# A fused attention and two-layer expert kernel: weights prepared once and kept in memory, gate column sums as products, low parts of x on two engines

## The chip, the cores and the metric

The kernel runs on one core of a Trainium2 chip. The core has a matrix engine (PE, with its weight loads shown apart as PEld), a vector engine (DVE), an activation engine (ACT), a general engine (POOL), and a queue engine (SP) that here issues every DMA. Each engine works through its own list of instructions in order; they meet only in semaphores. The metric is the device time of one execution in microseconds, lower is better.

## The reference, cut to what matters

```python
# 1: attention, 4 batches x 8 heads x 768 tokens x 64; each chunk of 32 queries sees its own
#    keys, 16 before, 8 behind and 8 memory keys        -> x: 3072 tokens x 512
# 2: first layer
a = x @ w_a                       # 512 -> 1536
b = x @ w_b
x = (a * b) @ w_out               # 1536 -> 512
# 3: gated experts, E = 8
logits = x @ w_gate
P = np.exp(logits - logits.max())
for _ in range(8):
    P /= P.sum(1, keepdims=True) + 1e-09      # rows: the 8 experts of one token
    P /= P.sum(0, keepdims=True) + 1e-09      # columns: all 3072 tokens of one expert
    P *= N / E
for e in range(E):
    h = np.maximum(x @ w1[e], 0.0)            # 512 -> 1024
    out += P[:, e:e+1] * (h @ w2[e])          # 1024 -> 512
```

All in float32. The kernel forms each float32 product of the two layers from three products of a coarse format (fp32r): every operand is split in a high part and a low part (what is left over).

## The kernel before, in words

**Stages.** Attention comes first. Then the first layer runs in 18 units (`v`, `M1 = 18`), and the expert layer in 96 units (`u`, `M2 = 96`). The tokens are cut into three pairs of token blocks (`PAIRS = 3`, 1024 tokens each). A pair takes `V1 = 6` units of the first layer or `V2 = 32` units of the expert layer, one unit for each slice of 256 hidden columns. So each weight slice is used by three units, one for each pair.

**A unit.** A chain is one "up" product x @ w for one slice; it is computed by a seven-product scheme on 2x2 blocks (`up(c, pos)`, pos 0 to 6, six matmuls each: two halves of the contraction times three high/low combinations). A unit of the first layer has two chains (w_a, w_b), a unit of the expert layer one. Between the up products PE works on the eight `down(w - 1, g)` groups, six matmuls each, of the unit before. So a unit of the first layer has 132 matmuls of 128x512, one of the expert layer 90.

**Weights.** For each unit SP loads a raw slice of 512 KB for each chain and one for down (`load_up`, `load_down`) into one of two slots of `raw`, as soon as the low parts of the slice before in that slot are done. POOL forms the sums of the scheme (`up_sums`, four instructions), ACT writes the high parts (`up_hi`, `down_hi`), POOL the low parts (`up_lo`, `down_lo`) into `W1` and `W2`, which have two buffers each. PE waits for the low parts (`w1_lo`, `w2_lo`) at pos 0 and at g 0. This is done again for every pair, 3 times for each slice.

**The operand x.** The seven left operands of a pair stand in `X`, one buffer. While the last chain of a pair runs, each is rebuilt for the next pair as its product gets done: `operand_sum` on DVE (four differences of 128x1024, in place in `Y`), `operand_hi` on ACT, `operand_lo` on POOL, in the order `X_BUILD`. There are five such changes of operand behind the first build: in units v = 5, v = 11, v = 17 (to the expert layer), u = 31 and u = 63. In the first layer POOL also forms the low parts of the hidden values (`g_lo`, four in each unit).

**The gate.** The logits of all tokens are collected in `gate` (128 x 24 x 8). The maximum and the eight rounds of the normalisation run in units u = 1 to 4: DVE does the row part and the column part (`sinkhorn_round`, `sinkhorn_columns`, each instruction waiting for the one before it, `link`), POOL adds over the partitions in between with `partition_all_reduce`. DVE runs three rounds in a row early in each of u = 2, 3, 4 (`sinkhorn_slot`), among its `accumulate` calls, which free the three PSUM banks of down (PE waits for `y_acc`). At the end of u = 4 `scale_first` multiplies the first expert's results by the gate.

The order on every engine is written out by hand. The code that the change touches:

## Time and profile before

| | us |
|---|---|
| median of 3 runs | 2885.74 (2880.82 to 2885.99) |
| the profiled execution, its device time | 2885.65 |
| its span, first to last instruction | 2883.9 |
| DVE busy | 1386.6 (48%) |
| ACT busy | 1051.4 (36%) |
| POOL busy | 1565.5 (54%) |
| DMA | 160.47 MB, mean 56 GB/s |

Times are in us unless marked ns. L12 is line 12 of the kernel. A row of the timeline gives start, duration, engine, line, operation, output <- inputs, count, and in brackets the idle time of that engine just before and what ended it ("issue": nothing that the profile shows). PEclk, the third number from the end in a row of a window, is the granted clock of PE as a share of 2.4 GHz; behind it stand the mean busy share of the 16 DMA engines and what they moved in GB/s. A busy PE is not a PE at its peak: at half the clock its matmuls last twice as long and it is still busy.

### The profile page before, as it was taken

How to read it: one execution, taken by the hardware profiler on the slowest of the kernel's cores; microseconds unless marked ns; L12 is line 12 of the kernel's file. 1: busy time of each engine (PE TensorE's matmuls, PEld its weight loads, DVE VectorE, ACT ScalarE, POOL GpSimd, SP SyncE). 2: the span in 40 equal slices, each digit the busy share in tenths (PEclk: the TensorE clock that was granted, in tenths of full speed). 3: DMA queues.
4: the chain of work that ended last, by engine and by line, in shares of the span. 5: the costliest groups of instructions: out<-in, count | busy, mean ns of one | idle time of the engine just before them, and what ended most of it. 6: DMA issues, size and time to landing. Idle time of an engine off the chain costs nothing.

```text
span 2883.9 us, 34150 instructions
## 1 busy us (share of the span) xinstructions
PE 2800.7 (97%) x12750; PEld 2263.1 (78%) x12750; DVE 1386.6 (48%) x1969; ACT 1051.4 (36%) x2149; POOL 1565.5 (54%) x1379
## 2 busy tenths in 40 slices
PE   9999989989986899999999999999999999999999
PEld 7877867867865788888887888888887888888887
DVE  4553343343355645444445545454545545454544
ACT  5664333333331233333333333333334333333332
POOL 3358786686773444454547445444547454454542
PEclk8989999999997999999999999999999999999999
DMA  7541111111110111111111211111111211111111
GB/s 133 118 95 47 58 41 46 52 44 45 52 44 29 44 47 56 45 59 45 59 45 55 77 51 52 48 56 45 58 44 52 81 52 52 51 52 49 54 45 51
DMA packets 196940, 160.47 MB, mean 56 GB/s; under 512 B 96944, under 2 KB 164528, under 8 KB 196784
## 3 DMA queue, kind: packets, MB, share of 16 engines
q1 hardware_dynamic: 196784, 158.38, 18.5%
q8 instruction: 99, 1.62, 0.2%
q14 instruction: 57, 0.47, 0.1%
HBM read 152.06 MB, written 6.29 MB: 55 GB/s over the span
## 4 chain that ended last, share of the span: by engine, by line
PE 90%; DVE 4%; POOL 3%; issue 3%; ACT 1%; DMA 0%; POOLq 0%; ACTq 0%; DVEq 0%
PE bank L536 41%; PE bank L603 41%; PE bank L476 2%; PE bank L498 2%; POOL X L383 1%; PE bank L487 1%; PE bank L472 1%; POOL W L372 1%; PE bank L456 1%; DVE Y L930 0%; PE bank L462 0%; POOL hid L402 0%; DVE Y L1056 0%; DVE Y L1002 0%; DVE Y L936 0%
## 5 line engine op out<-in xcount | busy, mean ns | idle before, releaser
L536 PE MATMUL bank<-X,W 128*128 128x512 f32 x5550 | 1430.3, 396 | 40.7 <-POOL X L383 20.4
L536 PEld LDWEIGHTS bank<-X,W 128*128 128x128 f32 x5550 | 1046.9, 189 | 295.7 <-POOL X L383 23.6
L603 PE MATMUL bank<-W,hid 128*128 128x512 f32 x4608 | 1176.0, 394 | 27.7 <-DVE Y L1002 26.7
L603 PEld LDWEIGHTS bank<-W,hid 128*128 128x128 f32 x4608 | 870.2, 189 | 227.1 <-DVE Y L1002 28.0
L999 DVE SCALAR_TENSOR_TENSOR Y<-bank,gate,Y 128x512 f32<-128x512 f32 x720 | 540.4, 751 | 607.2 <-PE bank L603 595.3
L377 POOL TENSOR_TENSOR W<-raw,W 128x1024 fp32r<-128x1024 f32 x114 | 276.0, 2421 | 541.5 <-ACT W L731 541.5
L372 POOL TENSOR_TENSOR W<-Ws,W 128x512 fp32r<-128x512 f32 x264 | 337.8, 1301 | 68.0 <-ACT W L723 68.0
L361 POOL TENSOR_TENSOR Ws<-raw 128x256 f32<-128x256 f32 x132 | 101.2, 767 | 358.4 <-DMA raw<-in_moe_w_dram 320.6
L372 POOL TENSOR_TENSOR W<-raw,W 128x512 fp32r<-128x512 f32 (+1 forms) x264 | 263.7, 1019 | 16.3 <-ACT W L723 16.3
L837 ACT ACTIVATE hid<-tmp 128x512 fp32r<-128x512 f32 x192 | 121.4, 632 | 400.7 <-DVE tmp L967 277.7
L603 PE MATMUL bank<-hid,W 128*128 128x512 f32 x864 | 225.3, 397 | 3.9 <-issue 3.8
L1102 DVE SCALAR_TENSOR_TENSOR hid<-bank,hid 128x512 fp32r<-128x512 f32 x192 | 132.7, 691 | 154.9 <-ACT hid L837 154.5
L781 ACT ACTIVATE tmp<-bank 128x512 f32<-128x512 f32 x132 | 78.5, 595 | 333.1 <-PE bank L536 333.0
L603 PEld LDWEIGHTS bank<-hid,W 128*128 128x128 f32 x864 | 164.7, 191 | 42.5 <-issue 5.6
L1002 DVE TENSOR_TENSOR Y<-Y,bank 128x512 f32<-128x512 f32 x144 | 98.7, 685 | 206.6 <-PE bank L603 206.3
L777 ACT ACTIVATE bank<-bank 128x512 f32<-128x512 f32 x131 | 76.2, 582 | 324.3 <-PE bank L536 324.3
L723 ACT ACTIVATE W<-Ws 128x512 fp32r<-128x512 f32 x264 | 151.1, 623 | 80.8 <-POOL Ws L366 80.8
L962 DVE TENSOR_TENSOR tmp<-bank,tmp 128x512 f32<-128x512 f32 x132 | 91.2, 691 | 180.3 <-ACT tmp L785 180.3
L837 ACT ACTIVATE hid<-bank 128x512 fp32r<-128x512 f32 x192 | 114.5, 596 | 164.5 <-PE bank L536 164.5
L785 ACT ACTIVATE tmp<-bank 128x512 f32<-128x512 f32 x132 | 78.8, 597 | 249.2 <-PE bank L536 249.2
L1102 DVE SCALAR_TENSOR_TENSOR hid<-tmp,hid 128x512 fp32r<-128x512 f32 x192 | 157.7, 821 | 5.3 <-ACT hid L837 1.7
L402 POOL TENSOR_TENSOR hid<-tmp,hid 128x512 fp32r<-128x512 f32 x72 | 97.8, 1361 | 99.8 <-ACT hid L791 99.2
(80 smaller groups left out, 1866.4 us busy)
## 6 DMA issues: line engine op xcount, KB each, us to landing
raw<-in_moe_w_dram SPq DMA_DIRECT2D x192, 512.0 KB, 3.4
raw<-in_moe_w_a_dram SPq DMA_DIRECT2D x18, 512.0 KB, 3.6
raw<-in_moe_w_b_dram SPq DMA_DIRECT2D x18, 512.0 KB, 3.5
raw<-in_moe_w_out_dram SPq DMA_DIRECT2D x18, 512.0 KB, 3.3
Kw<-in_k_dram SPq DMA_DIRECT2D x32, 240.0 KB
Vw<-in_v_dram SPq DMA_DIRECT2D x32, 240.0 KB
Qw<-in_q_dram SPq DMA_DIRECT2D x32, 192.0 KB
out_dram<-Y SPq DMA_DIRECT2D x24, 256.0 KB, 4.0
```

Source lines behind the costliest of these rows:

```text
L361: nc.gpsimd.tensor_tensor(s1, w_block(slot, 1, 0), w_block(slot, 1, 1), ALU.add).then_inc(w_sum, 1)
L372: nc.gpsimd.tensor_tensor(w_piece(c, n, 1), w_piece_of(slot, n), w_piece(c, n, 0).bitcast(F32), ALU.subtract).then_inc(w1_lo, 1)
L377: nc.gpsimd.tensor_tensor(W2[:, w % 2, 1, :], raw[:, item_w2(w) % 2, :], W2[:, w % 2, 0, :].bitcast(F32), ALU.subtract).then_inc(w2_lo, 1)
L402: nc.gpsimd.tensor_tensor(hid[:, v % 2, f, l, 1], g_of, hid[:, v % 2, f, l, 0].bitcast(F32), ALU.subtract).then_inc(f_lo, 1)
L536: last = nc.tensor.matmul(into[:, :], W1[:, c % 2, ws, w_slot, kc, :], X[:, pos, xs, kc, :], start=(start and kc == 0 and n == 0), stop=(k ...
L603: last = nc.tensor.matmul(into[:, :], lhsT, rhs, start=(j == 0 and n == 0), stop=(j == 1 and n == 2))
L723: nc.scalar.activation(w_piece(c, n, 0), w_piece_of(slot, n), ACT.Copy).then_inc(w1_hi, 1)
L837: nc.scalar.activation(hid[:, u % 2, f, l, 0], of, ACT.Relu).then_inc(e_hi, 1)
L962: nc.vector.tensor_tensor(into, bank[BANK_E][:, :], of, ALU.add).then_inc(c_22, 1)
L999: nc.vector.scalar_tensor_tensor(out=y, in0=ps, scalar=by, in1=y, op0=ALU.mult, op1=ALU.add).then_inc(y_acc, 1)
L1002: nc.vector.tensor_tensor(y, y, ps, ALU.add).then_inc(y_acc, 1)
L1102: nc.vector.scalar_tensor_tensor(out=hid[:, u % 2, f, l, 1], in0=of, scalar=0.0, in1=hid[:, u % 2, f, l, 0].bitcast(F32), op0=ALU.max, op1 ...
```

## The change

Weights: the units of the first pair of each layer (`fresh(w)`) prepare their weights as before, and SP stores the finished `W1` (1.84 MB) and `W2` (1.05 MB) buffers in two DRAM tensors (`keep_up`, `keep_down`). The units of the other two pairs load them from there straight into `W1` and `W2` (`fetch_up`, `fetch_down`). Of 36 + 96 chains 12 + 32 are still prepared.

```diff
+        w1_kept = nc.dram_tensor("w1_kept", [2 * V1 + V2, P, 4 * NP * P], F32).ap()
+        w2_kept = nc.dram_tensor("w2_kept", [V1 + V2, P, 4 * D], F32).ap()
+            def keep_up(c):
+                sp.wait_ge(w1_lo, 4 * (kept_w1(c) + 1))
+                sp.dma_start(w1_kept[kept_w1(c)], W1[:, c % 2]...).then_inc(s_w1s[c % 2], 16)
+            def keep_down(w):
+                sp.wait_ge(w2_lo, kept_w2(w) + 1)
+                sp.dma_start(w2_kept[kept_w2(w)], W2[:, w % 2]...).then_inc(s_w2s[w % 2], 16)
+            def fetch_up(c):
+                sp.wait_ge(p_prod, NP * (c - 1))
+                sp.wait_ge(s_w1s[c % 2], 16 * (V1 if c < C1 else V1 + V2 // 2))
+                sp.dma_start(W1[:, c % 2]..., w1_kept[kept_w1(c)]).then_inc(s_w1l[c % 2], 16)
+            def fetch_down(w):
+                sp.wait_ge(p_down, NG * (w - 1))
+                sp.wait_ge(s_w2s[w % 2], 16 * (V1 // 2 if w < M1 else V1 // 2 + V2 // 2))
+                sp.dma_start(W2[:, w % 2]..., w2_kept[kept_w2(w)]).then_inc(s_w2l[w % 2], 16)
             load_down(0)
-            for w in range(1, M1):
+            keep_up(0)
+            for w in range(1, V1):
                 load_up(2 * w)
+                keep_up(2 * w - 1)
                 load_up(2 * w + 1)
+                keep_down(w - 1)
                 load_down(w)
-            for u in range(M2):
+                keep_up(2 * w)
+            load_up(C1)
+            keep_up(2 * V1 - 1)
+            load_down(M1)
+            keep_down(V1 - 1)
+            for w in range(V1, M1):
+                fetch_up(2 * w)
+                fetch_up(2 * w + 1)
+                fetch_down(w)
+            keep_up(C1)
+            for u in range(1, V2):
                 load_up(C1 + u)
+                keep_down(M1 + u - 1)
                 load_down(M1 + u)
-                if u % V2 == 3 and u >= V2:
+                keep_up(C1 + u)
+            keep_down(M1 + V2 - 1)
+            for u in range(V2, M2):
+                fetch_up(C1 + u)
+                fetch_down(M1 + u)
+                if u % V2 == 3:
                     store(u // V2 - 1)
```

PE waits for `s_w1l`, `s_w2l` instead of `w1_lo`, `w2_lo` in those units. ACT's `up_hi` and `down_hi` wait also for the store of the buffer that they write over.

Low parts: DVE takes those of x for pos 3 and 5 and all of `g_lo`; POOL keeps pos 0, 1, 2, 4, 6. ACT's order of the high parts becomes 0, 1, 3, 2, 4, 5, 6. POOL's list is now: weights of v = 0 to 5, the three operand changes of the first layer with the weights of C1 before the third, weights of u = 0 to 31, two operand changes.

```diff
-X_BUILD = (0, 3, 1, 4, 2, 5, 6)
+X_POOL = (0, 1, 2, 4, 6)
+X_DVE = (3, 5)
+X_HI = (0, 1, 3, 2, 4, 5, 6)
+            def operand_lo(n, p, pos):                 # on DVE
+                dve.wait_ge(x_hi, NP * n + X_HI.index(pos) + 1)
+                nc.vector.tensor_tensor(X[:, pos, 1], x_source(p, pos), X[:, pos, 0].bitcast(F32),
+                                        ALU.subtract).then_inc(x_lo2, 1)
+            def g_lo(v, n, f, l):                      # on DVE
+                dve.wait_ge(f_hi, 4 * v + n + 1)
...
                 accumulate(v - 1, 4)                   # DVE, first layer
+                if n is not None:
+                    operand_sum(n, of, 1)
                 dve.wait_ge(f_a, 2 * v + 1)
                 dve.wait_ge(p_prod, NP * b + 4)
                 times(v, 0, bank[BANK_A][:, :])
+                if n is not None:
+                    operand_sum(n, of, 3)
                 accumulate(v - 1, 5)
-                    operand_sum(n, (p + 1) % PAIRS, 0)
-                    operand_sum(n, (p + 1) % PAIRS, 1)
+                g_lo(v, 0, 0, 0)
...
                 times(v, 2, bank[BANK_B][:, :])
+                g_lo(v, 1, 1, 1)
+                if n is not None:
+                    operand_sum(n, of, 2)
                 accumulate(v - 1, 7)
+                g_lo(v, 2, 0, 1)
                 sum_21(b, tmp[:, 4], tmp[:, 4])
                 dve.wait_ge(c_21, b + 1)
                 times(v, 3, tmp[:, 4])
...
-                    operand_sum(n, (p + 1) % PAIRS, 2)
-                    operand_sum(n, (p + 1) % PAIRS, 3)
+                    operand_lo(n, of, 3)
+                g_lo(v, 3, 1, 0)
+                if n is not None:
+                    operand_sum(n, of, 4)
+                    operand_lo(n, of, 5)
                 seed(c)                                # ACT, first layer, second chain
-                up_hi(c + 1)
+                if n is not None:
+                    operand_hi(n, of, 0, c)
+                if fresh(v + 1):
+                    up_hi(c + 1)
                 act.wait_ge(c_21, c)
                 copy_u(c, tmp[:, 4])
...
                 g_hi(v, 0, 0, 0)
+                if n is not None:
+                    operand_hi(n, of, 1, c)
                 act.wait_ge(c_22, c)
                 copy_v(c, tmp[:, 5])
...
                 g_hi(v, 3, 1, 0)
                 if n is not None:
-                    for x in range(3, NP):
-                        operand_hi(n, (p + 1) % PAIRS, x, c)
+                    operand_hi(n, of, 4, c)
+                    operand_hi(n, of, 5, c)
+                    operand_hi(n, of, 6, c)
```

Gate: the reductions over the partitions are products on PE into bank 6, a column of ones times the sums, and the maxima times a unit matrix. DVE's slots are spread over the unit, and PE takes the products after fixed groups of its own list. The column part has three instructions instead of four.

```diff
+            TOTALS = [(u, pos) for u in range(2, 6) for pos in (1, 3, 6)][1:1 + SINKHORN]
+            def total(n):
+                pe.wait_ge(g_one, 1)
+                pe.wait_ge(g_part, n + 1)
+                nc.tensor.matmul(b_sum[:, 0:E], one.to_broadcast([P, P]), col_s, start=True,
+                                 stop=True).then_inc(g_total, 1)
                     down(w - 1, pos)                   # PE, in the loop over pos
+                    if u == 1 and pos == 6:
+                        spread_maxima()
+                    if (u, pos) in TOTALS:
+                        total(TOTALS.index((u, pos)))
-                        nc.gpsimd.partition_all_reduce(col_t[:, :], col_s[:, :], P, RADD).then_inc(g_total, 1)
             def sinkhorn_columns(i):
-                dve.wait_ge(g_total, i + 1)
-                link(nc.vector.tensor_scalar(col_t[:, :], col_t[:, :], EPS, None, ALU.add))
-                link(nc.vector.reciprocal(col_t[:, :], col_t[:, :]))
-                link(nc.vector.tensor_scalar(col_t[:, :], col_t[:, :], float(N) / E, None, ALU.mult))
+                dve.wait_ge(g_total, i + 2)
+                link(nc.vector.tensor_scalar(col_t, b_sum[:, 0:E], EPS, float(E) / N, ALU.add, ALU.mult))
+                link(nc.vector.reciprocal(col_t, col_t))
                 link(nc.vector.tensor_tensor(by_expert, by_expert, ...))
+                slots = [3 * (u - 2) + g for g in range(3)] if u in (2, 3, 4) else [SINKHORN + 1] * 3
                 accumulate(w - 1, 0)
                 accumulate(w - 1, 1)
+                sinkhorn_slot(slots[0])
...
                 h_lo(u, 1, tmp[:, v_at], 1, 1)
+                sinkhorn_slot(slots[1])
...
                 accumulate(w - 1, 7)
+                sinkhorn_slot(slots[2])
```

## Rows read from the trace of the kernel before

**Rows 1.** The page: busy time, share and instructions of each engine.
```profile
PE 2800.7 (97%) x12750; PEld 2263.1 (78%) x12750; DVE 1386.6 (48%) x1969; ACT 1051.4 (36%) x2149; POOL 1565.5 (54%) x1379
```
**Rows 2.** Windows: from:to, length, busy of PE, PEld, DVE, ACT, POOL; PEclk, DMA, GB/s.
```profile
259.07:350.48 91.41, 91.41 (x397) 74.11 (x397) 32.73 (x48) 35.38 (x63) 66.73 (x63) 1.00 0.17 52
350.48:430.26 79.78, 67.69 (x265) 53.19 (x265) 32.68 (x36) 30.44 (x49) 64.14 (x50) 0.91 0.13 40
586.65:635.08 48.43, 36.99 (x133) 28.19 (x133) 22.30 (x20) 18.54 (x28) 41.51 (x29) 0.86 0.10 33
805.07:837.53 32.46, 23.19 (x91) 17.66 (x90) 20.23 (x19) 12.87 (x19) 29.23 (x18) 0.95 0.06 17
862.37:988.31 125.94, 94.32 (x361) 73.03 (x360) 78.22 (x139) 28.08 (x49) 48.16 (x49) 0.84 0.10 34
988.47:1506.64 518.17, 518.17 (x2252) 422.29 (x2251) 257.09 (x350) 176.52 (x300) 256.28 (x225) 1.00 0.16 51
1506.64:1553.30 46.66, 43.49 (x181) 34.69 (x181) 28.16 (x32) 20.45 (x31) 34.40 (x21) 0.96 0.11 34
2175.10:2221.81 46.71, 43.55 (x181) 34.77 (x181) 28.24 (x32) 20.45 (x31) 34.45 (x21) 0.96 0.10 34
```
**Rows 3.** Timeline of unit u = 2 and 3, where the gate is normalised.
```profile
890.64 0.43 POOL L444 PARTITION_ALL_REDUCE col_t<-col_s  x1 [6.80 <-issue]
891.10 0.17 DVE L1039 TENSOR_SCALAR col_t<-col_t 128x8 f32<-128x8 f32 x1 [19.57 <-POOL col_t L444]
894.03 0.68 DVE L1002 TENSOR_TENSOR Y<-Y,bank 128x512 f32<-128x512 f32 x1
894.22 0.40 POOL L444 PARTITION_ALL_REDUCE col_t<-col_s  x1 [3.15 <-DVE col_s L1035]
894.76 2.93 PE L603 MATMUL bank<-W,hid 128*128 128x512 f32 x6 [13.80 <-DVE Y L1002]
...
909.43 2.09 DVE L1039 TENSOR_SCALAR col_t<-col_t 128x8 f32<-128x8 f32 x1
917.46 0.69 DVE L1002 TENSOR_TENSOR Y<-Y,bank 128x512 f32<-128x512 f32 x1
```
**Rows 4.** Timeline of the same stretch, the fold of the logits.
```profile
857.32 0.95 PE L625 MATMUL bank<-fold,lg 128*128 128x8 f32 x8
```
**Rows 5.** Timeline of the operand change in v = 5, and one sum before it.
```profile
203.85 1.21 DVE L936 TENSOR_TENSOR Y<-Y 128x1024 f32<-128x1024 f32 x1
...
388.42 1.05 ACT L751 ACTIVATE X<-Y 128x1024 fp32r<-128x1024 f32 x1
...
390.42 2.41 POOL L383 TENSOR_TENSOR X<-Y,X 128x1024 fp32r<-128x1024 f32 x1
...
392.86 2.30 DVE L930 TENSOR_TENSOR Y<-Y 128x1024 f32<-128x1024 f32 x1 [1.56 <-POOL X L383]
...
395.19 3.27 DVE L933 TENSOR_TENSOR Y<-Y 128x1024 f32<-128x1024 f32 x1
...
413.73 5.49 PE L536 MATMUL bank<-X,W 128*128 128x512 f32 x12 [6.13 <-POOL X L383]
```
**Rows 6.** Timeline of one steady unit of the expert layer, its weights.
```profile
1077.17 2.42 POOL L377 TENSOR_TENSOR W<-raw,W 128x1024 fp32r<-128x1024 f32 x1 [6.08 <-ACT W L731]
...
1079.61 0.37 SPq L280 DMA_DIRECT2D raw<-in_moe_w_dram  x1
...
1084.91 0.37 SPq L273 DMA_DIRECT2D raw<-in_moe_w_dram  x1
...
1088.47 0.74 POOL L361 TENSOR_TENSOR Ws<-raw 128x256 f32<-128x256 f32 x1 [3.59 <-DMA raw<-in_moe_w_dram]
...
1091.13 0.74 POOL L366 TENSOR_TENSOR Ws<-raw,Ws 128x256 f32<-128x256 f32 x1
```
**Rows 7.** Windows: the attention stage; the stretch with eight output stores and two loads.
```profile
0.00:200.00 200.00, 195.72 (x1456) 157.46 (x1457) 99.05 (x203) 116.47 (x538) 77.93 (x91) 0.92 0.59 119
1583.30:1593.30 10.00, 10.00 (x45) 8.16 (x44) 4.97 (x7) 4.06 (x7) 3.44 (x4) 1.00 0.93 316
```

More of the change, by code:

```diff
@@ L113, in build @@
         b_lg, b_gate = bank[6], bank[7]
+        b_sum = bank[6]
         s_kq = [sem(f"s_kq{i}") for i in range(2)]
@@ L139, in build @@
         w2_lo = sem("w2_lo")
+        s_w1s = [sem(f"s_w1s{i}") for i in range(2)]
+        s_w2s = [sem(f"s_w2s{i}") for i in range(2)]
+        s_w1l = [sem(f"s_w1l{i}") for i in range(2)]
+        s_w2l = [sem(f"s_w2l{i}") for i in range(2)]
         x_sum = sem("x_sum")
@@ L207, in w_piece_of, with fresh, unit_of_chain, kept_w1 @@
             return Ws[:, 2 * n - 4:2 * n - 2].rearrange("p s c f -> p (s c) f")
+        def fresh(w):
+            return w < V1 or M1 <= w < M1 + V2
+        def unit_of_chain(c):
+            return c // 2 if c < C1 else M1 + c - C1
+        def kept_w1(c):
+            return c % (2 * V1) if c < C1 else 2 * V1 + (c - C1) % V2
+        def kept_w2(w):
+            return w % V1 if w < M1 else V1 + (w - M1) % V2
+        def loads_w1(c):
+            return sum(not fresh(unit_of_chain(i)) for i in range(c % 2, c + 1, 2))
+        def loads_w2(w):
+            return sum(not fresh(i) for i in range(w % 2, w + 1, 2))
         def item_w1(c):
-            return 3 * (c // 2) + c % 2 if c < C1 else 3 * M1 + 2 * (c - C1)
+            return 3 * (c // 2) + c % 2 if c < C1 else 3 * V1 + 2 * (c - C1)
         def item_w2(w):
-            return 3 * w + 2 if w < M1 else 3 * M1 + 2 * (w - M1) + 1
+            return 3 * w + 2 if w < M1 else 3 * V1 + 2 * (w - M1) + 1
         def unit_of(w):
@@ L396, in _ @@
                     up_lo(0)
-            operand_lo(0, 0, 6)
-            def g_lo(v, n, f, l):
-                pool.wait_ge(f_hi, 4 * v + n + 1)
-                g_of = tmp[:, n]
-                nc.gpsimd.tensor_tensor(hid[:, v % 2, f, l, 1], g_of, hid[:, v % 2, f, l, 0].bitcast(F32),
-                                        ALU.subtract).then_inc(f_lo, 1)
-            for v in range(M1):
-                p, i = unit_of(v)
+            operand_lo(0, 0, 4)
+            for v in range(V1):
                 up_sums(2 * v + 1)
@@ L542, in operands_ready @@
             def operands_ready(c, pos, n):
-                if pos == 0:
-                    pe.wait_ge(w1_lo, 4 * (c + 1))
-                if n is not None:
-                    pe.wait_ge(x_lo, NP * n + X_BUILD.index(pos) + 1)
+                if pos == 0 and fresh(unit_of_chain(c)):
+                    pe.wait_ge(w1_lo, 4 * (kept_w1(c) + 1))
+                elif pos == 0:
+                    pe.wait_ge(s_w1l[c % 2], 16 * loads_w1(c))
+                if n is not None and pos in X_POOL:
+                    pe.wait_ge(x_lo, len(X_POOL) * n + X_POOL.index(pos) + 1)
+                elif n is not None:
+                    pe.wait_ge(x_lo2, len(X_DVE) * n + X_DVE.index(pos) + 1)
             def up(c, pos, n):
@@ L581, in down @@
                 i = NG * w + g
-                if g == 0:
-                    pe.wait_ge(w2_lo, w + 1)
+                if g == 0 and fresh(w):
+                    pe.wait_ge(w2_lo, kept_w2(w) + 1)
+                elif g == 0:
+                    pe.wait_ge(s_w2l[w % 2], 16 * loads_w2(w))
                 if g % 4 == 0:
@@ L627, in gates_fold, with spread_maxima @@
                 last.then_inc(g_mm, 1)
+            def spread_maxima():
+                pe.wait_ge(g_max, 1)
+                nc.tensor.matmul(b_sum[:, 0:P], col_s[:, 0:1].to_broadcast([P, P]), ident[:, :],
+                                 start=True, stop=True).then_inc(g_total, 1)
+            def total(n):
[3 more added lines that the diff above has]
+                                 stop=True).then_inc(g_total, 1)
             pe.wait_ge(a_kt, R)
@@ L760, in _ @@
                 attention_step((B - 1) * G + g, g, G, ahead=(g < G - 1))
-                if g != 2:
-                    operand_hi(0, 0, (0, 1, 3, 4, 5, 6, 7).index(g), None)
                 if g == 2:
                     up_hi(0)
+                for pos in ((0,), (), (), (1,), (3,), (), (2, 4), (5, 6))[g]:
+                    operand_hi(0, 0, pos, None)
             for g in range(3):
@@ L798, in _ @@
                     seed(c)
-                up_hi(c + 1)
+                if fresh(v):
+                    up_hi(c + 1)
                 if v > 0:
@@ L807, in _ @@
                 copy_v(c, tmp[:, 5])
-                down_hi(v)
+                if fresh(v):
+                    down_hi(v)
                 act.wait_ge(p_prod, NP * c + 6)
@@ L863, in _ @@
                 copy_v(c, tmp[:, v_at])
-                if n is not None:
-                    operand_hi(n, p + 1, 2, c)
                 act.wait_ge(c_22, c + 1)
@@ L874, in _ @@
                 if n is not None:
-                    for x in range(4, NP):
-                        operand_hi(n, p + 1, x, c)
+                    operand_hi(n, p + 1, 4, c)
+                    operand_hi(n, p + 1, 5, c)
+                    operand_hi(n, p + 1, 6, c)
                 if u == 1:
```

225 lines of the change are left out of this document (114 added, 111 removed).

## The prediction

> **What bounds the kernel now.** I read the busy shares first [rows 1]. PE is busy 97% of the span and no other engine over 54%, so PE sets the end. What is not PE at its pace is little and has to be found, since a busy PE can run at half its clock.
>
> Then the windows [rows 2]. In 259.07 to 350.48 PE is busy 91.41 of 91.41 us: that is three units of the first layer (396 matmuls by count), 30.47 us each. In 988.47 to 1506.64 it is again fully busy: 25 units of the expert layer, 20.73 us each. Over most of the span there is therefore nothing to win by taking work off POOL, ACT or SP. The excess over these two paces stands in six places:
> - v = 5: 79.78 us for two units, 79.78 - 60.94 = 18.8.
> - v = 11: 48.43 for one, 18.0.
> - v = 17 into u = 0: the window runs from the last down group to the seventh one in u = 0, which at pace is two groups (2.76) and 17.97, together 20.73; 32.46 - 20.73 = 11.7.
> - u = 2 to 5: 125.94 for four, 125.94 - 82.92 = 43.0.
> - u = 31: 46.66 for two, 5.2, and u = 63: 46.71, 5.3.
>
> Together 102.0 us. In these windows the granted clock is 0.84 to 0.96, at pace 1.00: part of the excess is PE at the lower of its two levels (1.2 instead of 2.4 GHz) after it stood. Twelve matmuls took 5.49 us right after a stop of 6.13 [rows 5], where 12 x 0.230 = 2.8 is the pace.
>
> The timelines say what stands there. In the gate stage PE stops 13.80 us because DVE has not freed a bank, and DVE stands 19.57 us for POOL's reduction over partitions [rows 3]; of POOL's time before it 6.80 us have no releaser, and the next reduction comes 3.15 us after the last one's end with DVE's chain in between. In the operand changes a chain goes ACT high part 1.05, POOL low part 2.41, DVE sums [rows 5].
>
> **The change part by part.** The sum starts from the profiled execution, 2885.65 us (1.75 over its span, 0.1 under the median of the three runs). With all six places at pace it would be 2885.65 - 102.0 = 2783.6. What stays of each:
>
> *Gate.* The reductions leave POOL: the 13.80 and 19.57 us stops with the 6.80 without a releaser go. The new products: the fold of the logits makes four of the same kind in 0.95 us [rows 4], 0.24 each; nine are 2.1 us of PE. DVE's part of a round is 891.10 to 894.03, 2.9 us. A unit has 8 accumulates, 4 low parts and 2 sums at 0.68 to 0.75, about 10.2 us, plus three rounds 8.8: 19.0 of 20.73, so it fits. What is late next is PE's wait for `g_part`, behind which all of PE's list is queued. By DVE's order slot 1 ends about 18.3 us into the unit, PE takes its product at 19.3; slot 2 ends 4.7 us into the next, PE asks at 5.5. These margins are below a microsecond, and a round beside POOL's weight work is dear: from 909.43 to 917.46 it took 8.0 us instead of 2.9 [rows 3]. In the new kernel u = 2 to 4 are still units with fresh weights. One instruction of the five that can stand behind POOL is gone and one reads PSUM. Bounds: 0 to 2 us in each of four units if POOL is mostly elsewhere, 5 each if every slot is stretched and PE then drops its clock. I take 8 (u = 2: 1, u = 3 and 4: 2.5 each, and 2 for `scale_first`, whose eight products still stand before the next accumulates), plus 2.1 for the products: 10 stay of 43.
>
> *v = 5 and 11.* From the start of the unit, with a group of six at 1.38: the high part of pos 0 is done at 18.3, POOL is free (no weights, no `g_lo`), its low part 20.7, first sum 21.9 (1.21 alone, 2.30 and 3.27 beside POOL [rows 5]), second sum 24.1, high part of pos 1 25.1, the copy that product 5 waits for 25.7 against 26.3: in time. Before, `accumulate` and `times` stood ahead and POOL had weights first. But now DVE has, behind the last product's end at 30.4: low part 2 of hidden, sum_21, times, low part of pos 3, low part 3, sum 4. That is sum_21 at 31.3 to 32.9 where PE wants it at 31.8, and sum 4 at 36.4 alone or 38.9 beside POOL. ACT makes the high part of pos 6 behind it and only then the next chain's `seed`, 38.0 to 40.5, and PE wants that at 35.2. So PE stops 3 to 6 us and loses 0 to 2.5 of clock. I take 7 for each (3.5 to 12).
>
> *v = 17.* Here POOL has the four low parts of C1's weights before the low part of pos 0, which comes at about 25.9. DVE waits for it ahead of `times` 0, the first high part of hidden waits for `times`, and the copy for product 5, wanted at 26.3, stands behind it on ACT: 30.7. So 4.4 us of stop, 1.6 of clock, and then the same seed, 3.7 and 1.4: 11 stay of 11.7 (6 to 15). I expect nothing from the change here.
>
> *u = 31 and 63.* The same count with one chain: DVE's sum 1 at 8.9 instead of behind sum 22, product 5 in time, the seed 0.8 late, one bank 0.5 late: 2 and 1.5 stay (1 to 4 each).
>
> *`g_lo` on DVE.* Four instructions of 128x512, 0.68 each by the row of that size, make DVE 2.7 us of 30.47 busier in a unit of the first layer, whose window has it 36% busy. The one on a tight path, low part 2 ahead of sum_21, ends before the last product. I take 0 (up to 0.6 in each of the six units with POOL's weights, 4 us).
>
> *Weights kept.* In the units of pairs 2 and 3 the loads are 2.88 MB a unit. At the 316 GB/s of the stretch with eight stores [rows 7] that is 9.1 of 20.73 us; `fetch_up` is released a unit ahead. I take 0; without that cover PE would wait at pos 0. PE kept 10.00 of 10.00 us in that stretch, so the traffic itself costs it nothing. The Trainium skill (SBUF — State Buffer, "SBUF: two separate sides") says the same, that DMA and the engines don't share ports.
> In the first pair SP's queue gets the stores, and each `keep_up` is ahead of the next raw load with the same trigger. In the steady unit the load leaves at 1084.91, POOL starts its sums at 1088.47, 3.6 later, and ends them at 1091.87 [rows 6]; its next work is due at 1077.17 + 20.73 = 1097.90, so 6.0 us are spare. The store of 1.84 MB at 316 GB/s is 5.8. It just fits. Behind that, the low parts are ready 10 us before PE needs them (1084.91 is 10.8 us into a unit, by 988.47 as an anchor), so single delays don't count, only a cycle longer than 20.73. I take 0; the range is the rival below.
>
> *First build.* Two instructions more for ACT and POOL in the last two attention steps, one or two fewer before; the last normalising comes 2 us later but is not used until then. 0 (-1 to +2).
>
> Sum: 2783.6 + 10 + 7 + 7 + 11 + 2 + 1.5 = **2822 us**. Own bounds: 2800 to 2846.
>
> **The rivals.**
> *B, nearly all goes.* With POOL idle in v = 11, 17, u = 63 nothing contends, the sums are 1.21 and the stops stay under 2 us without a drop of clock: 13 us stay in all, 2797. For it: the uncontended sum of 1.21. Against it: ACT's order, high part 6 before `seed`, is a fact of the list.
>
> *C, DVE and POOL in turns.* Rows show that a sum is 1.21 alone and 2.30 to 3.27 beside POOL, a round 2.9 and 8.0. If this holds wherever both are at work, low parts on two engines run one after the other, and moving pos 3 and 5 gains 2 x (2.41 - 1.21) only. Then the changes of operand keep 12, 12, 15, 4, 4, and the gate 20: 2783.6 + 67 = 2851. The Trainium skill (SBUF — State Buffer, "Who interferes with whom") states such a rule, an instruction of DVE with two SBUF inputs and one of POOL that reads SBUF exclude each other for the whole instruction; the sum of 1.21 against 2.30 agrees. Against its full price: in v = 11, 17 and u = 63 POOL has almost nothing but its five low parts.
>
> *D and E, the weights of the first pair become the bound.* The loop is: low parts done, store 1.84 MB and raw load, sums 3.4, low parts of down and up 7.7 less 0.8 of waiting. The transfers may take 10.4 us; they take 3.56 + 1.84/r, plus 1.57/r - 5.3 where the W2 store and load of 1079.61 are not yet through. That is binding below r = 285 GB/s. At 245: 12.2, 1.8 us in each of 31 units less the 10 in hand, +45: 2867 (D). E, on the other side: at the attention stage's rate, 119 GB/s at a busy share of 0.59, 202 at full, it is 15.1, 4.7 x 31 - 10 = 137: 2959. It is slower than before from +64, that is below some 235 GB/s. For it: the margin is 10%, and nothing in the trace shows a large store. Against it: eight stores in a row with two loads moved 316 GB/s at a share of 0.93, and packets of 14 KB a row should be no worse than 2 KB. The Trainium skill (DMA: Bandwidth & Descriptors, "Bandwidth") has 341 GB/s for a transfer of 1 MB; by it the store is 5.4 us and fits.
>
> **How the numbers follow.** Forecast 0.58, B 0.13, C 0.12, D 0.07, E 0.08, and 0.02 that the gains and costs cancel. The time is the forecast's, 2822. The range runs from just under B to D, 2794 to 2868; E, the cancelled case and the ends of B and D are left out. Faster by over 0.2% (5.8 us, about what a measurement of this kernel tells from no change): 0.90, within 0.2%: 0.02, slower: 0.08.
>
> **What would show it.** In the profile after: POOL's busy time falls by more than half, from 1565.5 to about 600, and DVE's rises by some 50; windows of u = 2 to 5 with 8 to 12 us over pace; v = 5 and 11 with a stop of PE of 3 to 6 us released by ACT's seed (bank<-bank), v = 17 with two such stops; no partition reduction; steady units still 30.47 and 20.73 in all three pairs. Wrong, if units of the first expert pair are longer than those of the second (D, E), if stops at the operand changes are released by POOL's or DVE's low parts of x, or if PE in u = 3 or 4 stops for DVE's column sums by over 5 us.

## The result, and the profile after

The changed kernel takes 2807.68 us (median of 4 runs, 2801.41 to 2820.09) against 2885.86 (4 runs, 2880.82 to 2912.06): 0.9717 of the time, 95% interval 0.9649 to 0.9784. (The medians include the profiled execution; the ratios here and below are not those of the medians, and differ from them by up to 0.002.) The forecast was 2822, the range 2794 to 2868. In a second timing of six runs it was 2804.18 (2799.80 to 2809.13), 0.9708 (0.9681 to 0.9735). The profiled execution took 2808.93 us, 2.1 over its span.

The page's busy times, with which [rows 1] compare:

```profile
span 2806.8 us, 32949 instructions
PE 2769.6 (99%) x12768; PEld 2253.9 (80%) x12768; DVE 1420.4 (51%) x2047; ACT 816.9 (29%) x1721; POOL 580.4 (21%) x506
```
POOL's busy time falls by 985 us and ACT's by 235, and that by itself gives nothing. PE has the same matmuls and is busy 31 us less too: most of that is busy time that was spent at the lower clock (twelve matmuls in 5.49 us instead of 2.8 [rows 5]), some 5 are the two paces, which are a little shorter.

The windows of the changed kernel, same columns as [rows 2]:

```profile
376.44:415.26 38.82, 33.62 (x133) 26.73 (x133) 24.57 (x26) 13.94 (x19) 13.88 (x5) 0.91 0.46 180
415.26:570.62 155.36, 155.36 (x693) 126.16 (x693) 68.33 (x102) 36.03 (x60) 0.00 (x0) 1.00 0.41 152
570.62:608.03 37.41, 32.17 (x134) 25.71 (x133) 24.58 (x26) 13.94 (x19) 16.71 (x9) 0.95 0.34 127
808.34:920.70 112.36, 110.34 (x502) 88.58 (x501) 80.53 (x149) 35.82 (x61) 51.57 (x46) 1.00 0.57 198
920.70:1438.37 517.67, 517.67 (x2252) 422.97 (x2251) 255.69 (x350) 176.68 (x300) 255.11 (x225) 1.00 0.55 190
1438.37:1481.26 42.89, 41.67 (x181) 33.72 (x181) 29.35 (x34) 16.21 (x22) 15.17 (x6) 1.00 0.35 135
1481.26:2102.45 621.19, 621.19 (x2701) 507.60 (x2701) 301.65 (x420) 127.19 (x210) 0.00 (x0) 1.00 0.36 143
```
Row 1 and 3 each hold one unit's time and the stops of one change (v = 5 and 11): 8.6 and 7.2 us over the first layer's pace, which is now 30.24. Row 2 is five units with 4.2 us of products for the logits. Row 4 holds u = 1 to 5, 8.8 over 5 x 20.71, of which 4.4 is u = 1 (the logits, 4.1 before too). Row 5 and 7 are the steady units of pair 1, with stores (190 GB/s), and of pair 2, with loads alone: 20.71 each. Row 6 is u = 31.

The waits of PE by what ended them: total, times, longest.

```profile
PE bank L593 <- ACT bank L857: 12.9, 5, 3.9
PE bank L593 <- ACT tmp L865: 5.6, 3, 4.1
PE bank L593 <- DVE tmp L1063: 4.0, 3, 1.4
PE bank L666 <- DVE Y L1096: 1.2, 1, 1.2
PE bank L701 <- DVE lg L1136: 0.8, 1, 0.8
```
L857 is `seed`, L865 the copy that product 5 waits for, L1063 `sum_21`, L1096 an `accumulate`, L1136 DVE's column sums. Of POOL only the identity matrix at the launch's start is left in the list (2.1 us), neither the reduction nor a low part of X.

### The profile page after: what moved, and what is told of

Same layout as the page of the kernel before. It is cut to its first block, busy times and chain, and to the rows that moved or that the text cites. A ratio compares the mean times of both kernels' runs of the same rounds, so it can differ in the third digit from the quotient of the medians.

```text
span 2806.8 us, 32949 instructions
## 1 busy us (share of the span) xinstructions
PE 2769.6 (99%) x12768; PEld 2253.9 (80%) x12768; DVE 1420.4 (51%) x2047; ACT 816.9 (29%) x1721; POOL 580.4 (21%) x506
## 4 chain that ended last, share of the span: by engine, by line
PE 93%; DVE 4%; ACT 1%; issue 1%; POOL 0%; DVEq 0%; ACTq 0%; POOLq 0%
PE bank L593 44%; PE bank L666 43%; PE bank L530 2%; PE bank L552 2%; PE bank L541 1%; PE bank L526 1%; DVE tmp L1066 1%; PE bank L510 0%; DVE Y L1027 0%; DVE X L1031 0%; PE bank L516 0%; DVE Y L1157 0%; ACT Pr L775 0%; DVE Y L1099 0%; DVE hid L1217 0%
## 5 line engine op out<-in xcount | busy, mean ns | idle before, releaser
L1096 DVE SCALAR_TENSOR_TENSOR Y<-bank,gate,Y 128x512 f32<-128x512 f32 x720 | 539.7, 750 | 592.2 <-PE bank L666 580.8
L457 POOL TENSOR_TENSOR X<-Y,X 128x1024 fp32r<-128x1024 f32 x30 | 79.0, 2640 | 868.9 <-ACT X L831 868.8
L1058 DVE TENSOR_TENSOR tmp<-bank,tmp 128x512 f32<-128x512 f32 x132 | 91.3, 691 | 171.9 <-ACT tmp L865 171.9
L857 ACT ACTIVATE bank<-bank 128x512 f32<-128x512 f32 x131 | 76.2, 582 | 322.3 <-PE bank L593 322.3
L865 ACT ACTIVATE tmp<-bank 128x512 f32<-128x512 f32 x132 | 78.8, 597 | 262.2 <-PE bank L593 262.2
L1217 DVE SCALAR_TENSOR_TENSOR hid<-tmp,hid 128x512 fp32r<-128x512 f32 x192 | 142.1, 740 | 5.2 <-ACT hid L923 0.7
L446 POOL TENSOR_TENSOR W<-raw,W 128x512 fp32r<-128x512 f32 x88 | 88.4, 1026 | 206.0 <-ACT W L803 206.0
L1063 DVE TENSOR_TENSOR tmp<-bank,tmp 128x512 f32<-128x512 f32 x132 | 91.2, 691 | 72.5 <-PE bank L593 71.3
L446 POOL TENSOR_TENSOR W<-Ws,W 128x512 fp32r<-128x512 f32 x88 | 112.9, 1305 | 23.5 <-ACT W L803 23.5
L775 ACT ACTIVATE Pr<-bank,nmax 96x128 f32<-96x128 f32 x256 | 89.6, 358 | 73.1 <-DVE nmax L978 73.0
L451 POOL TENSOR_TENSOR W<-raw,W 128x1024 fp32r<-128x1024 f32 x38 | 91.7, 2413 | 73.1 <-ACT W L812 73.1
```

What stands on the lines that cost most here:

```text
L446: nc.gpsimd.tensor_tensor(w_piece(c, n, 1), w_piece_of(slot, n), w_piece(c, n, 0).bitcast(F32), ALU.subtract).then_inc(w1_lo, 1)
L451: nc.gpsimd.tensor_tensor(W2[:, w % 2, 1, :], raw[:, item_w2(w) % 2, :], W2[:, w % 2, 0, :].bitcast(F32), ALU.subtract).then_inc(w2_lo, 1)
L457: nc.gpsimd.tensor_tensor(X[:, pos, 1], x_source(p, pos), X[:, pos, 0].bitcast(F32), ALU.subtract).then_inc(x_lo, 1)
L775: last = nc.scalar.activation(Pr[0:QT, g % 4, f, j, :], b_s[f][0:QT, j * P:(j + 1) * P], ACT.Exp, bias=nmax[0:QT, f, j:j + 1], accum_out=e ...
L1058: nc.vector.tensor_tensor(into, bank[BANK_E][:, :], of, ALU.add).then_inc(c_22, 1)
L1063: nc.vector.tensor_tensor(into, bank[BANK_E][:, :], of, ALU.add).then_inc(c_21, 1)
```

## The experiments

Each was run beside the kernel before, and its ratio is to that. "Over pace" is read in the profiled execution from the starts of the units, the first product of one to the first of the next; a change of operand in unit v is felt in v and v + 1, and "the change in v = 5" is the sum of both. The edits are shortened to their main lines.

**1. The gate part alone**: the kernel before with `col_t` and `col_s` as products with ones, spread over slots; weights and low parts as before.

```diff
-            nc.gpsimd.partition_all_reduce(col_t, col_s, ...)
+            nc.tensor.matmul(b_sum[:, 0:E], one.to_broadcast([P, P]), col_s, ...)   # eight rounds, u = 2 to 4
```


> The kernel before with the gate part of the change alone: reductions over the partitions as products on PE, the rounds spread over the units; weights, operand builds and low parts as before. My theory is that the parts add up and the gate's is the largest: the stage keeps about 5 us over pace instead of 43, so 2886 - 38 = 2848 (2842 to 2854). Rival: the short gate stage of the changed kernel needs the other parts too, because POOL here gets its raw weights earlier and works beside DVE's rounds, which are then stretched as the 8.0 us round before; then 10 to 15 us stay, 2856 to 2862.

2845.50 us (2843.58 to 2848.89), 0.9851 (0.9828 to 0.9874), as expected. Units u = 2 to 5 are 6.7 us over pace, 43.0 before; the operand changes stay (18.1, 18.1, 11.8, 5.2 and 5.3).

**2. Stored weights alone**: gate and low parts as before.

```diff
-            for w in range(1, M1): load_up, load_up, load_down
+            for w in range(1, V1): load_up, keep_up, load_up, keep_down, load_down, keep_up
+            for w in range(V1, M1): fetch_up, fetch_up, fetch_down
```


> The kernel before with the stored weights alone; gate, order of the builds and low parts as before. Theory: steady units are at PE's pace with or without it, so the gain can only come at the operand changes where POOL no longer has weights ahead of the low parts (v = 11, u = 63): 0 to 12 us, 2874 to 2886. Rival: taking 1000 us of work off POOL is what made the kernel faster, 30 us or more: under 2856. Second rival: the added traffic costs something, over 2890.

2868.05 us (2864.84 to 2870.85), 0.9928 (0.9904 to 0.9952): 6 below the range, the gain is larger than expected. The unit starts show where. The change in v = 5 costs 13.5 us over pace instead of 18.8, that in v = 11 12.6 instead of 18.0, the gate units 39.5 instead of 43.0. At pace nothing moved in the expert layer (20.727 us a unit in both).

**3. No stored weights**: the changed kernel with every unit preparing its own. Stores and fetches are gone, and POOL's low parts of X stand behind the next unit's weights.

```diff
-            return w < V1 or M1 <= w < M1 + V2
+            return True
```


> The changed kernel without the stored weights: every unit prepares its own, gate and builds as changed, POOL's low parts of x behind the next unit's weights (in the expert layer pos 0 ahead of them). Theory: v = 5 and v = 11 now look like v = 17, where the low part of pos 0 comes behind four weight instructions: 10 us each instead of 8.6 and 7.2, and u = 31 and 63 a microsecond or two more; 2809 + 4 to 12 = 2813 to 2821. Rival (stored weights are the main gain): over 2840.

2829.17 us (2825.12 to 2842.47), 0.9804 (0.9766 to 0.9841): 8 above the range. Its v = 5, timeline:

```profile
386.52 2.40 POOL L442 TENSOR_TENSOR X<-Y,X 128x1024 fp32r<-128x1024 f32 x1
388.95 1.23 DVE L998 TENSOR_TENSOR Y<-Y 128x1024 f32<-128x1024 f32 x1 [5.59 <-POOL X L442]
393.60 2.55 PE L576 MATMUL bank<-X,W 128*128 128x512 f32 x6 [4.08 <-ACT tmp L846]
407.82 4.54 PE L576 MATMUL bank<-X,W 128*128 128x512 f32 x12 [3.87 <-ACT bank L838]
416.26 1.62 PE L576 MATMUL bank<-X,W 128*128 128x512 f32 x6 [2.55 <-ACT tmp L842]
```
The unit starts at 363.24. POOL, busy with weights, gives the first low part of X 25.7 us into it, and DVE has stood 5.59 us for that. So PE stops 4.08 for the copy of product 5 (L846), the stop that the prediction put in v = 17 alone; in v = 6 the seed's 3.87 (L838) comes on top, and 2.55 for the copy that product 4 waits for (L842). Against the changed kernel the change in v = 5 is 6.1 us dearer, that in v = 11 7.5, the gate 5.1, u = 31 and 63 together 5.2: 23.9 in all.

**4. The seed first**: the changed kernel with `seed` of the next chain ahead of the high parts of X that DVE's last sum releases.

```diff
                     operand_hi(n, of, 2, c)
+                    seed(c + 1)
                 g_hi(v, 3, 1, 0)
```


> The changed kernel with one thing moved on ACT: at the five operand changes the seed of the next chain is issued before the high parts that DVE's last sum holds up (first layer: ahead of the fourth high part of hidden and pos 4, 5, 6; expert layer: ahead of pos 5 and 6). Theory: the stops of PE for the seed (12.9 us in five places) and the lower clock behind them go: v = 5 and 11 keep about 2 instead of 8.6 and 7.2, v = 17 6 instead of 10.4, u = 31 and 63 about 0.5: 2809 - 17 = 2792 (2788 to 2797). Rival: the next in ACT's list, the copy for product 4, stands behind high part 6 and takes the seed's place: less than half of it, 2800 to 2806.

2794.16 us (2785.33 to 2806.77), 0.9666 (0.9639 to 0.9693). v = 6, where the stop of the change in v = 5 falls by this count, goes from 8.6 us over pace to 2.2, v = 12 from 7.2 to 2.2, u = 32 and 64 from 1.4 each to 0.2. No wait on `seed` is left in the list. That ACT's order, not the amount of work, holds those stops is shown. One place missed: v = 17 and u = 0 keep 9.7 us of 10.5 where 6 was expected, and PE's waits for the copy of product 5 rise from 5.6 us to 8.0; part of the seed's stop seems to go over to the copy there.

**5. Stores twice**: in the first expert pair each up part is stored a second time, to memory that nobody reads.

```diff
                 keep_up(C1 + u)
+                keep_again(C1 + u)
```


> The changed kernel with each finished W1 buffer of the first expert pair (u = 1 to 31) stored a second time, to another tensor, between its store and the next raw load: 1.84 MB more ahead of that load, nothing else. Theory (the weights' loop): the raw load now lands 8.2 us after its trigger, the loop allows 10.4; with the second store about 12.9, so each unit is 2.5 us longer, 30 units less the 10 us in hand: +65, 2874 (2855 to 2900), with units of 23 us in the first expert pair and 20.71 in the second. Rival: the transfer engines have a busy share of 0.55 there, so the load still lands in time: +0 to 8.

2870.86 us (2862.45 to 2883.05), 0.9949 (0.9930 to 0.9969). POOL in two steady units of that pair:

```profile
1019.07 0.73 POOL L443 TENSOR_TENSOR Ws<-raw 128x256 f32<-128x256 f32 x1 [12.66 <-DMA raw<-in_moe_w_dram]
...
1042.58 0.73 POOL L443 TENSOR_TENSOR Ws<-raw 128x256 f32<-128x256 f32 x1 [13.32 <-DMA raw<-in_moe_w_dram]
```
The cycle is 23.5 us here, 23.07 in the mean over the pair's steady units, 20.71 in the next pair. The count said 10.4 us may pass from the low parts to the landing; 12.7 to 13.3 pass, 2.3 to 2.9 too many. In the changed kernel it is 8.24:

```profile
1004.57 0.74 POOL L435 TENSOR_TENSOR Ws<-raw 128x256 f32<-128x256 f32 x1 [8.24 <-DMA raw<-in_moe_w_dram]
```
So rivals D and E were built on the right loop, which has 2.2 us of room, and failed on the rate. (By its own terms the loop binds below 281 GB/s, not 285.)

**6. Low parts of X at the changes back on POOL**: pos 3 and 5 of every build but the first.

```diff
-                    operand_lo(n, of, 3)       # DVE; and 5
+                    for i in range(NP): operand_lo(n, p, i)   # POOL
```


> The changed kernel with the low parts of pos 3 and 5 back on POOL at the five operand changes (in the first build they stay on DVE). Theory: the two engines exclude each other when both have two SBUF inputs, DVE's pos 5 took 3.37 us instead of 1.21 there, so the split saves nothing: within 3 us of the changed kernel, 2806 to 2812, perhaps a microsecond less at each change in the first layer because the sum before high part 6 comes earlier. Rival: two engines at work are what shortened the changes: 3 to 5 us more at each in the first layer, 2820 to 2826.

2807.25 us (2802.67 to 2822.80), 0.9737 (0.9692 to 0.9782), as expected: no difference from the changed kernel. v = 6 is 6.7 over pace instead of 8.6, u = 0 6.9 instead of 4.6; all changes of operand together keep 30.5 us, 29.2 in the changed kernel. The split of the second to sixth build has no gain, once `g_lo` and the weights have left POOL.

**7. Rounds in a row**: the three rounds of a unit in successive slots instead of spread.

```diff
-            TOTALS = [(u, pos) for u in range(2, 6) for pos in (1, 3, 6)][1:1 + SINKHORN]
+            TOTALS = [(u, pos) for u in range(2, 6) for pos in (0, 1, 2)][1:1 + SINKHORN]
```


> The changed kernel with DVE's rounds again one behind the other early in u = 2, 3, 4 (behind accumulate 0, 1 and 2) and PE taking their products behind down groups 0, 1 and 2 of the next slots. Theory: both the reduction's place and the spreading count; PE stands 1 to 3 us for most sums and DVE's list runs behind: the stage keeps 15 to 25 us instead of 4.7, 2819 to 2829. Rival: the partition reductions on POOL were all of it, and the order among the accumulates is worth nothing: 2807 to 2811.

2812.72 us (2807.29 to 2816.02), 0.9749 (0.9717 to 0.9780). PE's waits:

```profile
PE bank L701 <- DVE lg L1136: 7.7, 5, 2.7
```
The gate units are 12.3 us over pace, 4.4 in the changed kernel. Both count, as the theory had it, but the stage keeps less than the expected 15 to 25 and the median lies 6 below the range: 8 us are the spreading's, some 31 come with the reductions on PE (and one instruction less in each column part).

**8. Three moves at once**: the seed first, POOL's low part of pos 0 in v = 17 ahead of the weights of C1, and DVE's low part of pos 5 in the first build after the last attention step.

```diff
             up_sums(C1)
+            operand_lo(3, 0, 0)
             up_lo(C1)
```


> The changed kernel with three moves: the seed first as in the run before, POOL's low part of pos 0 in v = 17 ahead of the low parts of C1's weights, and DVE's low part of pos 5 in the first build behind the last two attention steps. Theory: the first is worth 17, the second takes the 4.1 us stop with its lower clock out of v = 17 (4 to 6), the third the wait of PE for DVE's copies at the end of the attention, where that low part took 4.70 us (2 to 4): 2809 - 25 = 2784 (2779 to 2792). Rival: at the changes the stops move to the next instruction in line, under half of it: 2797 or more.

2784.50 us (2780.01 to 2802.09), 0.9642 (0.9609 to 0.9674), as expected, and the fastest of all. v = 17 is 0.5 over pace (5.9 in the changed kernel), u = 0 5.5 instead of 4.6: the copy's 4.1 us stop is gone, part of it is late one chain on. The two units keep 6.0 together, 9.7 with the seed's move alone. The third move brought little: PE's second stop for a copy of PT is 0.32 us instead of 1.46, and from the first up group to v = 1 it takes 32.2 us, against 32.0 in experiment 4.

**9. First build on POOL**: the changed kernel with all seven low parts of the first build POOL's.

```diff
-                if g == 0:
-                    operand_lo(0, 0, 5)        # DVE, and 3
+            operand_lo(0, 0, 5); operand_lo(0, 0, 6)   # POOL, all seven
```


> The changed kernel, but in the first build of X (last attention steps) all seven low parts are POOL's again; the other builds stay split. Theory (the split of the first build is what moved the start of v = 1 from 244.57 to 239.95 us, because POOL's low parts delay `normalise` and PE, once it stands, runs at half its clock near 190 to 220 us): v = 1 starts 4 to 7 us later than in a run of the changed kernel whose clock dip at the launch's start is the same, a stretch at a granted clock of 0.50 stands between 180 and 220 us, and the median is 2811 to 2815. Rival (the dip there is chance, or comes with the order of DVE's sums): v = 1 starts where it does in the changed kernel, clock 1.00 from 180 to 210, median 2806 to 2809.

2815.06 us (2808.99 to 2825.89), 0.9742 (0.9713 to 0.9771), against 2804.18 of the run below in the same comparison. The number looks like the theory's, and the profile contradicts it: the granted clock is 1.00 in every window from 160 to 240 us, and from the first up group to v = 1 it takes 32.5 us, which lies between the 31.7 and 32.9 of the two profiles of the changed kernel. What is later is the launch's start. A window of this kernel, then of the changed one:

```profile
40.00:60.00 20.00, 20.00 (x91) 15.81 (x91) 6.23 (x13) 7.71 (x36) 4.07 (x4) 0.50 0.27 59
```
```profile
40.00:60.00 20.00, 20.00 (x166) 16.12 (x166) 10.50 (x23) 11.83 (x56) 6.87 (x7) 1.00 0.90 177
```
Both are code that the change doesn't touch. Its runs at a mean clock of 0.992 took 2808.99 to 2810.46 us, those of the changed kernel at 0.992 to 0.993 2807.19 to 2809.13: some 2 us are the edit's. The rival is nearer to the truth, though its median was missed by 6.

**10. The changed kernel again.**

> The changed kernel once more, beside the one above on the same chip: 2803 to 2812 us. From its profile: the granted clock of 0 to 60 us sets by how much its first group of up products may be compared with that of the other.

2804.18 us. Three runs at a mean clock of 0.992 to 0.993 took 2807.19 to 2809.13, three at 0.996 2799.80 to 2801.18.

## Why the prediction was right, and where its terms were off

Each term against the profiled execution after, in us over pace:

| term | before | forecast | after |
|---|---|---|---|
| gate, u = 2 to 5 | 43.0 | 10 | 4.4 |
| v = 5 | 18.8 | 7 | 8.6 |
| v = 11 | 18.0 | 7 | 7.2 |
| v = 17 and u = 0 | 11.7 | 11 | 10.5 |
| u = 31 | 5.2 | 2 | 1.5 |
| u = 63 | 5.3 | 1.5 | 1.4 |
| before v = 2 | | 0 | -3.6 |
| the two paces | | 0 | -5.0 |

2783.6 + 33.6 - 3.6 - 5.0 = 2808.6, measured 2808.93. The forecast was 13 too high: 5.6 by the gate, 8.6 by two terms that it set to 0, and 1 back from the rest. The mechanism was right at all five changes of operand and at the gate; that the sum of places fits to 0.3 us is in part luck, since the two profiled executions happen to have an equally long start at the lower clock, and its length moves the start of the first up group by up to 20 us between others (see the end).

*v = 5, 11, 17.* The mechanism is as written. Timeline of v = 5 after:

```profile
394.93 2.37 POOL L457 TENSOR_TENSOR X<-Y,X 128x1024 fp32r<-128x1024 f32 x1 [4.71 <-ACT X L831]
395.54 2.31 DVE L1066 TENSOR_TENSOR tmp<-tmp 128x512 f32<-128x512 f32 x1
395.65 1.63 PE L593 MATMUL bank<-X,W 128*128 128x512 f32 x6 [1.36 <-DVE tmp L1063]
399.51 1.21 DVE L1027 TENSOR_TENSOR Y<-Y 128x1024 f32<-128x1024 f32 x1
399.54 6.70 POOL L457 TENSOR_TENSOR X<-Y,X 128x1024 fp32r<-128x1024 f32 x2 [2.24 <-ACT X L831]
400.65 3.37 DVE L1031 TENSOR_TENSOR X<-Y,X 128x1024 fp32r<-128x1024 f32 x1
400.82 1.06 ACT L831 ACTIVATE X<-Y 128x1024 fp32r<-128x1024 f32 x1 [0.40 <-DVE Y L1027]
401.78 0.58 ACT L857 ACTIVATE bank<-bank 128x512 f32<-128x512 f32 x1
402.50 5.46 PE L593 MATMUL bank<-X,W 128*128 128x512 f32 x12 [3.84 <-ACT bank L857]
```
DVE's last sum (L1027) ends at 400.7, ACT makes the high part of pos 6 behind it and only then the seed at 401.78; PE stops 3.84 and runs the next twelve in 5.46 instead of 2.8. The forecast had stop 3 to 6 and 0 to 2.5 of clock. DVE's low part takes 3.37 where the same two-input form took 1.21 elsewhere, POOL's two take 6.70 for 4.7: the two engines hold each other up, as in [rows 5], though POOL had nothing else to do. The Trainium skill (SBUF — State Buffer, "Who interferes with whom") says that a DVE instruction with two SBUF inputs contends with one of POOL that reads SBUF; the trace agrees. That was rival C's mechanism, and experiment 6 has its answer: two engines gain nothing here. Its time was 43 us too long, of which 15.6 are the gate (it kept 20, 4.4 were left), 17.8 the changes (47 against 29.2), and the rest the terms that the forecast had missed too. v = 17 has both stops that were counted, 4.1 forecast 4.4, and 2.8 forecast 3.7:

```profile
779.84 2.20 PE L593 MATMUL bank<-X,W 128*128 128x512 f32 x6 [4.08 <-ACT tmp L865]
794.09 2.66 PE L593 MATMUL bank<-X,W 128*128 128x512 f32 x6 [2.77 <-ACT bank L857]
```

*Gate: the mis-sized term.* It charged stretched rounds in u = 3 and 4 with 2.5 each and took the nine products as 2.1 of PE. A product (one row, two matmuls in the trace) puts the next group off by 0.14 us, eight of them 1.1, and in the whole stage PE stops twice:

```profile
885.24 0.28 PE L701 MATMUL bank<-lg 128*128 128x8 f32 x2
885.38 1.63 PE L593 MATMUL bank<-X,W 128*128 128x512 f32 x6
...
863.73 0.36 PE L701 MATMUL bank<-lg 128*128 128x8 f32 x2 [0.81 <-DVE lg L1136]
903.33 7.97 DVE L1157 TENSOR_SCALAR Y<-Y,gate 128x512 f32<-128x512 f32 x8
912.14 1.66 PE L666 MATMUL bank<-W,hid 128*128 128x512 f32 x6 [1.21 <-DVE Y L1096]
```
The forecast took POOL's weight work at its old place in the unit. The raw load now waits for the store, and POOL's sums start 4.6 us later. Of the eight rounds only one meets a low part of the weights, and that is PE's 0.81 us stop:

```profile
860.44 2.40 POOL L451 TENSOR_TENSOR W<-raw,W 128x1024 fp32r<-128x1024 f32 x1 [1.80 <-ACT W L812]
860.52 2.53 DVE L1134 TENSOR_TENSOR gate<-gate,lg 128x192 f32<-128x192 f32 x1
```
In the other rounds this instruction takes 0.36. With no store, in experiment 3, two rounds meet one (2.14 and 2.43 us), the second with a dearer stop:

```profile
896.42 2.43 DVE L1113 TENSOR_SCALAR lg<-lg 128x24 f32<-128x24 f32 x1
...
900.93 0.36 PE L684 MATMUL bank<-lg 128*128 128x8 f32 x2 [2.04 <-DVE lg L1117]
```
POOL's low part there runs from 896.41 to 898.82, and DVE's instruction on 128x24 ends with it, at 898.85. Experiment 3's four gate units are 9.5 us over pace, near the forecast's 10, those of experiment 1, also without stores, 6.7. So the forecast priced stretched rounds as they come without the store, which moved them; of the 5.1 us more in experiment 3, though, 2.3 fall in u = 4 with that stop and 2.9 in u = 5, behind `scale_first`.

*Weights kept.* Traffic cost nothing, as said: 20.71 in all three pairs. The prediction had POOL free in v = 5 and 11 because of them, and was right. The expectations for experiments 2 and 3 then gave the stored weights too little, by 6 and 8 us at the ends of their ranges, for they took them to be worth little at the changes: without them the first low part of X is late in v = 5 and 11 as it is in v = 17. POOL's order at the four changes makes 18.8 of the 23.9 us of experiment 3, the gate the rest.

*First build: the step that failed.* It was set to 0 (-1 to +2) by counting the instructions that move, with no wait behind them. PE reaches the first up group at 207.07 instead of 215.39, 8.3 us earlier, behind an equally long slow start; v = 1 starts 4.6 us earlier and v = 2 3.6. In the kernel before, POOL has a low part of X ahead of its normalising in six of the last eight attention steps, and one of them falls in the step in which DVE forms two sums of 128x1024:

```profile
179.11 3.32 POOL L383 TENSOR_TENSOR X<-Y,X 128x1024 fp32r<-128x1024 f32 x1
180.75 1.71 DVE L904 TENSOR_SCALAR rsum<-esum 96x8 f32<-96x8 f32 x1
183.18 0.94 PE L498 MATMUL bank<-PT,Vw 128*64 128x96 f32 x8 [0.88 <-DVE PT L898]
```
DVE's instruction on 96x8 takes 1.71 us and ends with POOL's low part, the copy of PT behind it is late, and PE stops 0.88 us. In the changed kernel POOL has no low part in that step and the instruction takes its usual 0.15:

```profile
180.38 0.15 DVE L991 TENSOR_SCALAR rsum<-esum 96x8 f32<-96x8 f32 x1
```
All three kernels with the old build (before, 1 and 2) have this stop of 0.88, none with a new one has it. In the kernel before PE is at its lower level behind it: eight products of scores take 2.02 us at 184.64, 1.11 in the changed kernel. The four attention steps up to the last one take, from one step's first score product to the next's, 7.1, 11.2, 8.7 and 6.1 us in the kernel before; in both experiments with the old build (1 and 2) the four make 28.3 and 29.8, in the changed kernel, its repeat and experiments 3 to 8 25.2: 6.3, 6.1, 6.7, 6.1. Experiments 1 and 2 have a second such place three steps later: DVE's sum takes 3.49 and 3.23 us beside a low part of POOL (1.21 alone), PE stops 1.50 and 0.70, or 0.42 and 0.70, and is at its lower level again behind it, in experiment 1 for the first time. Experiments 1 and 3 differ in the low parts and the order of the builds alone, share the length of their slow start, and reach v = 1 at 247.29 and 240.67. Windows of the kernel before, and then of the changed one:

```profile
180.00:191.00 11.00, 10.12 (x57) 7.67 (x55) 6.96 (x13) 7.37 (x30) 7.70 (x7) 0.68 0.43 90
191.00:200.00 9.00, 9.00 (x43) 7.33 (x43) 2.21 (x5) 3.85 (x18) 6.52 (x7) 0.50 0.24 53
```
```profile
180.00:191.00 11.00, 10.91 (x89) 8.66 (x88) 6.70 (x15) 9.21 (x38) 7.67 (x8) 1.00 0.62 132
191.00:200.00 9.00, 8.45 (x70) 6.74 (x69) 8.93 (x14) 4.41 (x22) 5.43 (x5) 1.00 0.21 49
```
Experiment 9 puts all seven on POOL without that stretch coming back (its four steps make 26.3), but in four steps instead of six, and none in the step of the two sums; the one beside DVE's third sum costs a stop of 0.70. So not how much POOL has, but beside what it has it fits what was seen. That is read from the traces, not shown by a run: one with the old placing in the new kernel was not made, and that DVE's last sum comes one step later, in experiment 9 too, is a rival that no run excludes. Why the clock fell behind the 0.88 us stop in two kernels and not in experiment 1 is open.

The change gives 3.7 us back from there to v = 1. Two copies of PT that PE waits for 0.32 each before come later by 1.40 and 1.46: the first because DVE's 96x8 instruction stands 2.88 us beside two low parts of POOL (it is there in experiments 8 and 9 too), the second because DVE's low part of pos 5 takes 4.70 us at 212.07 (in experiments 8 and 9, without it there, 0.32).

*Paces.* 0.23 us in each of some 14 units of the first layer and 0.02 in each of some 90 expert units. In the former 0.15 is a short stop of PE at product 4 of the first chain: the copy that it waits for stood on ACT behind high parts of the weights, these behind POOL's sums, these behind `g_lo`. It is gone where the weights are fetched (30.32 in experiment 2's later units) and where `g_lo` is DVE's (30.24 in experiment 3, though it prepares all weights). The other 0.08 is open. The latter comes with the gate part (20.707 in experiment 1, 20.727 in 2); by what is open.

*By parts.* Gate alone -1.5%, stored weights alone -0.7%, together with the low parts -2.8%. From experiment 1 to 3, which adds the low parts and the order of the builds, 16 us go; from 3 to the changed kernel, which adds the stored weights, 21 to 25.

## What to carry to other kernels

Where one engine is busy nearly all the time, take the excess over the steady pace place by place, and name for each the last instruction in the list of the engine that releases it. Ask what stands ahead of that instruction: putting one instruction of 0.6 us two to four places forward at five changes gained 14 us, nearly as much as the 16 of moving all of `g_lo` and two low parts of every build to another engine. When a transfer is put before a load, work out anew where in the unit the work that waits for the load will fall.

## What the runs showed of the hardware that was not expected

- The start of the launch varies by execution, in code common to all kernels. Windows from 20 to 40 us stand at a granted clock from 0.50 to 1.00; of the attention steps of 6.1 us none takes 11.1 at half clock in experiments 5 and 7, two do in 4 and 8, three in 9. With the new build the first up group starts at 200.1 to 220.3 accordingly, 226.3 in experiment 9. Within one kernel the runs spread by 5 to 22 us and go with their mean granted clock (2801.41 at 0.996, 2820.09 at 0.989); that the start makes most of this is inferred, since only one execution of each has a trace. So differences below 10 us are to be read from places, not from two profiles' spans.
- Storing 1792 KB and loading 512 KB behind it was done 8.24 us after the low parts, 286 GB/s for the 2.36 MB as one with all delays in it. In between the 16 DMA engines moved 403 GB/s for 4 us, so the 316 of [rows 7] is no ceiling. A window of the changed kernel, and the page's line on the store with its median of 6.7 us from issue to landing:

```profile
997.00:1001.00 4.00, 4.00 (x19) 3.29 (x18) 2.54 (x4) 1.43 (x3) 0.00 (x0) 1.00 1.03 403
w_kept<-W SPq DMA_DIRECT2D x44, 1792.0 KB, 6.7
```
- A short stop can cost more than itself or nothing more: 0.88 us at 183.2 in the kernel before was followed by some 17 us at half clock, the same stop in experiment 1 (0.88 at 185.0) by none, and 1.36 us at 395.65 in the changed kernel by a group of six at 1.63 us, which is its full rate.
- Not only large instructions of DVE are stretched beside POOL: ones on 96x8 and 128x24 with one tensor as input took 1.4 to 3.1 us instead of 0.15 to 0.18.
